# Expert stage of an attention, gated feed-forward and routed-expert kernel: order of the first row turnings, the second gather and the weight splits

## The chip, the cores and the metric

The program runs on one core of a Trainium2 chip, as one launch. The metric is device time in microseconds; lower is better. A profiled execution has a span (first to last instruction) and, a little longer, a time of its own.

## What is computed

Three stages follow one another. Attention makes an array of 1792 tokens x 768 features. A gated feed-forward (`moe_`) maps each token to `(sigmoid(x @ w_gate) * (x @ w_val)) @ w_out`. Then every token goes to one of 8 experts:

```
logits = x @ w_gate                      # 1792 x 8
e_idx = argmax(logits, axis=1)
gate_w = softmax(logits)[n, e_idx]
eom = sigmoid(x @ w_output_gate)
for e in range(8):
    mask = e_idx == e
    h = maximum(x[mask] @ w1[e], 0)      # 768 -> 1024
    out[mask] = gate_w * eom[:, e] * (h @ w2[e])   # 1024 -> 768
```

With these inputs the experts get 254, 262, 211, 264, 216, 255, 174 and 156 tokens, that is 2, 3, 2, 3, 2, 2, 2 and 2 tiles of up to 128 rows: 18 expert tiles, numbered g = 0 to 17. The first tiles of experts 1 to 7 are g = 2, 5, 7, 10, 12, 14 and 16.

## The kernel before

All products are made from 16-bit halves: each number is split into a high part and a low part (the rest), and a product is three passes (high x high, high x low, low x high). ScalarE makes the high part of a weight piece (`split_high`, L815), VectorE the low part (`split_low`, L1042), SyncE loads the raw piece. An expert has 14 pieces: p = 0 to 5 are `w1` (128 x 1024, 512 KB), p = 6 to 13 are `w2` (128 x 768, 384 KB). `w_hi_ready` and `w_lo_ready` count the pieces. Raw pieces go through 7 stage buffers (`stage`), and each load waits until the low part of the piece that used the buffer before has been made; expert 0 has 3 buffers of its own for its first pieces. Split `w1` and `w2` have two homes, for odd and even experts.

**Token stage.** `down(t, s, fs)` (L1449) makes the second product of the feed-forward for token tile t (14 tiles, 12 chunks f, 3 passes, 2 halves of 384 columns: 72 multiplications a tile). ScalarE and VectorE (`y_high` L802, `y_low` L1069) turn the sum into high and low parts, and SyncE stores them to HBM (`store_y`). The routing (L1107 to L1217 on VectorE) runs beside the last two tiles. While it lasts, expert 0's pieces 0 to 5 are split ahead of the first token tile.

**Expert stage.** For tile g GpSimd gathers 128 rows from HBM (`gather`, L602) and TensorE turns them (`turn_rows`, L1493, 12 transposes); VectorE copies them to `x_t` (`rows_out`, L1229). Per tile, TensorE's queue is: the first half of the up product (`up`, b = 0, L1506, 18 multiplications), the 16 transposes of the previous tile's hidden layer (`turn_hidden`, L1515), the second half of `up`, `turn_rows(g + 1)`, and the down product of the previous tile (`rows_down`, L1528, 48 multiplications). ScalarE takes the hidden sums out of PSUM (L848), VectorE splits them (L1244, L1246) and copies the turned hidden layer (`turned_hidden`, L1234); the down product waits for this copy. `rows_done` (L835, ScalarE) weights the result rows and `scatter` (L615) writes them out. Engines take their queues strictly in order and meet at semaphores; the order is written out by hand in `tile(e, s, before, first)` of each engine, where `before` is g - 1 and `first` marks an expert's first tile.

The splits of the next expert's weights stand in the first tile of an expert. ScalarE makes three pieces ahead of that tile's hidden sums, three between them, and the eight `w2` pieces after them. Expert 1 has a catch-up of its own in g = 2. At the seam, `turn_rows(0)` stands behind the last `down`, and GpSimd, after all token tiles are stored, first clears `out_rows`, sends one scatter that writes no row, and then gathers for g = 1.

## Time and profile before

| | us |
|---|---|
| median of 3 runs | 1143.47 |
| lowest and highest run | 1142.17 and 1146.43 |
| profiled execution, its time | 1139.88 |
| profiled execution, its span | 1138.1 |
| TensorE busy | 1100.3 (97% of the span) |
| VectorE, ScalarE, GpSimd busy | 594.7, 425.9, 256.5 |

The token stage's first product starts at 633.22 us of the span, the expert stage's at 804.89, and the last multiplication ends at about 1129.5. The time of the profiled execution lies 3.6 below the median, so differences are added to either, and never an absolute time of the span to the median.

### The profile page before, as it was taken

Reading aid. Unit: us, or ns where it says so; the run is one execution under the profiler, and the core shown is the slowest. Engines: PE = TensorE matmul, PEld = TensorE weight load, DVE = VectorE, ACT = ScalarE, POOL = GpSimd, SP = SyncE. Lnnn points to the kernel's source line nnn. Section 1 sums busy time; section 2 is a strip of 40 time slices with the busy share of each in tenths; the row PEclk is TensorE's granted clock in tenths of the full one; section 3 lists DMA queues with packets and bytes.
Section 4 is the critical chain, followed back from the end, with each engine's and each line's share of the span. In section 5 each row is a group of like instructions: output and inputs, shape, how many; then the busy total and the mean of one; then the engine's idle time right before and its main releaser. Section 6 shows DMA issues by size and latency. Waiting matters only on the chain.

```text
span 1138.1 us, 17823 instructions
## 1 busy us (share of the span) xinstructions
PE 1100.3 (97%) x6617; PEld 573.3 (50%) x6618; DVE 594.7 (52%) x837; ACT 425.9 (37%) x631; POOL 256.5 (23%) x235
## 2 busy tenths in 40 slices
PE   7989999999999999999999999999898999999996
PEld 3434444444455555555555555556454555555554
DVE  7888888887433443333343300015656565556721
ACT  5768777777511111211111200001535253353510
POOL 4756767672200000000000000000211122112211
PEclk9999999999999999999999999999899999999999
DMA  5412222210121111111100501000848355366400
GB/s 144 122 49 62 61 65 58 66 25 17 60 67 56 56 55 55 55 55 55 55 28 1 195 28 41 28 32 23 296 163 319 118 211 206 108 217 225 142 20 18
DMA packets 71978, 104.11 MB, mean 91 GB/s; under 512 B 29310, under 2 KB 47870, under 8 KB 71920
## 3 DMA queue, kind: packets, MB, share of 16 engines
q1 hardware_dynamic: 63680, 89.84, 24.0%
q0 software_dynamic: 3120, 11.02, 2.7%
q10 hardware_dynamic: 5120, 2.48, 0.8%
q8 instruction: 36, 0.59, 0.2%
q14 instruction: 22, 0.18, 0.0%
HBM read 93.88 MB, written 13.76 MB: 95 GB/s over the span
## 4 chain that ended last, share of the span: by engine, by line
PE 87%; ACT 4%; DVE 4%; issue 2%; DMA 2%; ACTq 0%; POOL 0%; DVEq 0%; POOLq 0%; SPq 0%
PE ps L1434 29%; PE ps L1449 15%; PE ps L1528 12%; PE ps L1357 10%; PE ps L1506 7%; PE ps L1336 5%; PE ps L1316 2%; ACT arena L815 2%; DVE arena L1042 2%; PE ps L1348 2%; PE ps L1299 2%; PE ps L1338 1%; DMA arena<-in_moe_w 1%; PE ps L1515 1%; PE ps L1493 1%
## 5 line engine op out<-in xcount | busy, mean ns | idle before, releaser
L1434 PE MATMUL ps<-arena 128*128 128x448 f16 x1728 | 328.8, 352 | 0.0
L1434 PEld LDWEIGHTS ps<-arena 128*128 128x128 f16 x1728 | 168.1, 98 | 155.7
L1449 PE MATMUL ps<-arena 128*128 128x392 f16 (+1 forms) x1008 | 167.3, 329 | 2.4 <-DVE arena L1022 2.4
L1506 PE MATMUL ps<-arena 128*128 128x512 f16 x648 | 150.5, 388 | 5.6 <-DVE arena L1229 5.6
L1042 DVE SCALAR_TENSOR_TENSOR arena<-arena 128x768 f16<-128x768 f32 (+1 forms) x112 | 113.1, 1066 | 74.1 <-ACT arena L815 74.0
L1528 PE MATMUL ps<-arena 128*128 128x384 f16 x864 | 143.3, 326 | 4.0 <-DVE arena L1234 3.6
L1449 PEld LDWEIGHTS ps<-arena 128*128 (+1 forms) x1008 | 98.4, 98 | 70.4 <-DVE arena L1022 2.8
L1357 PE MATMUL ps<-arena 128*128 128x448 f32 x288 | 133.0, 573 | 0.0
L785 ACT ACTIVATE arena<-ps 128x448 f32<-128x448 f32 x48 | 26.1, 543 | 263.0 <-PE ps L1434 263.0
L1016 DVE SCALAR_TENSOR_TENSOR arena<-ps,arena 128x448 f32<-128x448 f32 x48 | 30.0, 624 | 176.0 <-PE ps L1434 96.1
L1528 PEld LDWEIGHTS ps<-arena 128*128 128x128 f16 x864 | 83.5, 98 | 58.6 <-issue 2.5
L940 DVE TENSOR_REDUCE arena<-ps 112x2 f16<-112x896 f32 x96 | 99.2, 1076 | 18.6 <-PE ps L1316 18.5
L815 ACT ACTIVATE arena<-arena 128x768 f16<-128x768 f32 (+1 forms) x112 | 97.5, 929 | 27.6 <-DMA arena<-in_moe_w 23.7
L1506 PEld LDWEIGHTS ps<-arena 128*128 128x128 f16 x648 | 63.7, 100 | 80.1 <-DVE arena L1229 6.4
L712 ACT ACTIVATE arena<-ps,arena 128x896 f32<-128x896 f32 x72 | 72.5, 1007 | 33.3 <-PE ps L1338 33.3
L960 DVE RECIPROCAL arena<-arena 128x448 f32<-128x448 f32 x24 | 70.8, 2951 | 10.3 <-ACT arena L730 10.3
L1336 PE MATMUL ps<-arena 64*128 64x448 f16 (+1 forms) x576 | 72.0, 356 | 3.0 <-ACT arena L712 1.7
L620 POOL MEMSET arena<- 128x1536 f16 x1 | 1.4, 1377 | 324.1 <-PE ps L1434 324.1
L835 ACT ACTIVATE arena<-ps,arena 128x384 f32<-128x384 f32 x36 | 18.9, 576 | 141.4 <-PE ps L1528 141.4
L1357 PEld LDWEIGHTS ps<-arena 128*128 128x128 f32 x288 | 47.6, 191 | 45.5 <-issue 45.5
L802 ACT ACTIVATE arena<-ps 128x768 f16<-128x768 f32 x14 | 11.3, 810 | 144.0 <-PE ps L1449 144.0
L1076 DVE TENSOR_SCALAR arena<-ps 128x16 f32 (+1 forms) x12 | 2.1, 171 | 119.9 <-ACT arena L802 119.9
(170 smaller groups left out, 1078.7 us busy)
## 6 DMA issues: line engine op xcount, KB each, us to landing
arena<-in_moe_w SPq DMA_DIRECT2D x48, 512.0 KB, 6.3
arena<-in_moe_w SPq DMA_DIRECT2D x64, 384.0 KB, 3.9
arena<-in_qk SPq DMA_DIRECT2D x23, 448.0 KB, 3.5
y_parts<-arena SPq DMA_DIRECT2D x16, 384.0 KB, 2.3
arena<-in_v SPq DMA_DIRECT2D x48, 96.0 KB, 2.6
arena<-in_moe_w_out SPq DMA_DIRECT2D x12, 384.0 KB, 5.5
arena<-in_w_out_t SPq DMA_DIRECT2D x11, 384.0 KB, 3.1
arena<-in_moe_w_gate SPq DMA_DIRECT2D x10, 384.0 KB, 4.2
```

The source lines that it names most:

```text
L712: nc.scalar.activation(probs[n % 2][:, :, i - 1], ps_pair(SCORE_SLOT, 128), ACT.Exp, bias=lift[:, 1:2])\
L815: nc.scalar.activation(hi, raw_rows(e, p), ACT.Copy, scale=S_OP).then_inc(w_hi_ready, 1)
L940: nc.vector.tensor_reduce(neg_max[n % 2][:, :, j], ps_pair(max_slot(n, j)), AX_X, ALU.max, negate=True)\
L960: nc.vector.reciprocal(sums_inv[n % 2], sums[n % 2]).then_inc(sums_inv_ready, 1)
L1016: nc.vector.scalar_tensor_tensor(gated[b % 2], ps[:, 2 * (b % 2) + 1, 0:S], 1.0 / S_OP, gate[b % 2], ALU.mult, ALU.mult).then_inc(gated_re ...
L1042: nc.vector.scalar_tensor_tensor(lo, raw_rows(e, p), S_OP, hi, ALU.mult, ALU.subtract).then_inc(w_lo_ready, 1)
L1336: nc.tensor.matmul(outs[h], qk_t[n % 3][rows, 1, kl, ks], qk_t[n % 3][rows, 0, ql], start=(kl + ql == 0), stop=False)
L1357: last = nc.tensor.matmul(ps[:, 6 + h, SQ], v_ones[n % 3][:, c, h * D:h * D + 2 * D], probs[n % 2][:, h, c], start=False, stop=(c == KCH - 1))
L1434: last = nc.tensor.matmul(ps[:, 2 * (b % 2) + g, 0:S], up_w[s][:, g, c, wl], xt[:, b * KC + c, xl], start=(c == 0 and wl + xl == 0), stop= ...
L1449: last = nc.tensor.matmul(ps[:, 4 + 2 * s + h, 0:cols], gt[:, f, gl, bass.ds(t * 128, 128)], wo[:, f, wl, h, 0:cols], start=(f == 0 and gl ...
L1506: last = nc.tensor.matmul(ps[:, b, :], x_t[:, xl, c], w1_s[s][:, c, wl, b * 512:(b + 1) * 512], start=(c == 0 and xl + wl == 0), stop=(c = ...
L1528: last = nc.tensor.matmul(ps[:, 4 + h, 0:HALF_DM], hid_t[:, b, hl, c], w2_s[s][:, k, wl, h * HALF_DM:(h + 1) * HALF_DM], start=(k == 0 and ...
```

## The change

Five things are reordered, and nothing that is computed changes.

1. Seam: the last two chunks of the last `down` are made half by half (`down_half`), and `turn_rows(0)` stands between the halves. ScalarE and VectorE take the halves out one by one, and VectorE's `rows_out(0)` stands ahead of both.
2. GpSimd reads the register that says which stores to wait for earlier, and gathers for g = 1 ahead of the clearing.
3. Weight splits: `w2` pieces of an expert e are split in e's own first tile, four ahead of the hidden sums and four between them, and `w1` of e + 1 behind them. Expert 0's pieces 0 to 10 are split between token tiles, 11 to 13 in g = 0, and expert 1's `w1` in g = 0 (three before, three after the second hidden sum). VectorE's `turned_hidden` of the previous tile now stands behind four low parts of 768 columns, where it stood behind three of 1024.
4. Raw pieces: expert 0 has 2 and then 4 buffers in memory that the feed-forward's first product and its weights have left. Expert 1's fourth load waits until the gather for g = 1 has landed.
5. End: the last down product makes its left half of columns in full and then the right one, in PSUM banks 0 and 1, and each half is weighted and scattered by itself, with indices of half rows.

```diff
@@ SyncE @@
+            sp.wait_ge(gt_lo_ready, B * FC)
+            sp.wait_ge(wo_lo_ready, FC)
...
-            sp.wait_ge(y_sum, TT)
+            sp.wait_ge(y_sum, TT + 1)
             def load_expert(e, s):
-                for p in range(KC + EARLY_STAGES if is_at(e, 0) else 0, PIECES):
+                for p in range(PIECES):
+                    if is_at(e, 1) and p == 3:
+                        sp.wait_ge(gathered, 32)
                     if p >= STAGES:
...
+                        sp.wait_ge(w_lo_ready, PIECES * e + p - STAGES + 1)
+                    elif not is_at(e, 1):
+                        sp.wait_ge(w_lo_ready, PIECES * (e - 1) + p + STAGES + 1)
@@ GpSimd @@
-            pool.wait_ge(route, ROUTE_ROWS)
+            pool.wait_ge(route, ROUTE_FIRST)
             tiles = pool.value_load(counts_i[0:1, 2 * E + 2:2 * E + 3], min_val=2, max_val=TT)
...
+            pool.wait_ge(route, ROUTE_ROWS)
+            pool.wait_ge(y_stored[0], even)
+            pool.wait_ge(y_stored[1], odd)
             gather(0)
             pool.wait_ge(route, ROUTE_DONE)
-            for s in range(2):
-                pool.wait_ge(y_stored[s], 8 * TT)
+            gather(1)
             nc.gpsimd.memset(out_rows, 0.0).then_inc(empty_ready, 1)
...
-            gather(1)
...
-            scatter(last)
+            for h in range(2):
+                cols = slice(h * HALF_DM, (h + 1) * HALF_DM)
+                pool.wait_ge(half_idx_ready, 2)
+                pool.wait_ge(out_ready, rows[h])
+                nc.gpsimd.indirect_dma_start(out=out.rearrange("n (h d) -> (n h) d", h=2),
...
@@ ScalarE @@
-            split_high(0, 0, range(KC))
-            over_token_tiles(act, y_high)
+            split_high(0, 0, (0, 1))
+            y_high(0, 0)
+            split_high(0, 0, (2, 3))
+            y_high(1, 1)
+            split_high(0, 0, (4, 5))
+            y_high(2, 0)
+            split_high(0, 0, range(KC, KC + 4))
+            y_high(3, 1)
+            split_high(0, 0, (KC + 4,))
+            over_token_tiles(act, y_high, 4)
...
             def tile(e, s, before, first):
                 g = before + 1
...
+                if first:
+                    split_high(e, s, range(KC + 5, PIECES) if is_at(g, 0) else range(KC, KC + 4))
+                hidden(g, 0)
                 if is_at(g, 0):
-                    split_high(e + 1, 1 - s, range(KC))
-                else:
+                    split_high(e + 1, 1 - s, range(0, 3))
+                elif first:
+                    split_high(e, s, range(KC + 4, PIECES))
+                hidden(g, 1)
+                if first and not is_at(e, E - 1):
+                    split_high(e + 1, 1 - s, range(3 if is_at(g, 0) else 0, KC))
+                if not is_at(g, 0):
                     rows_done(before)
@@ VectorE @@
             rows_out(0)
-            split_low(0, 0, range(KC, PIECES))
+            for h in range(2):
+                cols = slice(h * HALF_DM, (h + 1) * HALF_DM)
+                dve.wait_ge(y_hi_ready, TT + h)
+                nc.vector.scalar_tensor_tensor(y_parts[1][:, 1, cols], ps[:, 6 + h, 0:HALF_DM], 1.0 / S_OP, y_parts[1][:, 0, cols],
+                                               ALU.mult, ALU.subtract).then_inc(y_lo_ready, 1)
...
+                if first:
+                    split_low(e, s, range(KC + 5, PIECES) if is_at(g, 0) else range(KC, KC + 4))
                 if not is_at(g, 0):
                     turned_hidden(before, 0)
                     turned_hidden(before, 1)
                 hidden_split(g, 0)
...
+                if is_at(g, 0):
+                    split_low(e + 1, 1 - s, range(0, 3))
+                elif first:
+                    split_low(e, s, range(KC + 4, PIECES))
                 rows_out(g + 1)
...
                 hidden_split(g, 1)
...
+                if first and not is_at(e, E - 1):
+                    split_low(e + 1, 1 - s, range(3 if is_at(g, 0) else 0, KC))
@@ TensorE @@
+            def down_half(h):
+                for f in range(FC - 2, FC):
+                    for gl, wl in PASSES:
+                        last = nc.tensor.matmul(ps[:, 6 + h, 0:HALF_DM], gt[:, f, gl, (TT - 1) * 128:TT * 128],
+                                                wo[:, f, wl, h, 0:HALF_DM], start=False, stop=(f == FC - 1 and gl == 1))
+                last.then_inc(y_sum, 1)
+            down(TT - 1, 1, range(4, FC - 2))
+            down_half(0)
             pe.wait_ge(route, ROUTE_DONE)
             turn_rows(0)
+            down_half(1)
             over_experts(pe, tile)
             last = last_tile(pe)
             turn_hidden(last, 0)
             turn_hidden(last, 1)
-            pe.wait_ge(out_ready, 2 * last)
-            rows_down(E - 1, 1, last)
```

TensorE at the seam, before, from the routing table's product to the turning of g = 1:

```order
L1481 MATMUL ps<-arena 128x110 x14
L1449 MATMUL ps<-arena 128x384 x48
L1493 MATMUL ps<-arena 128x128 x12
L386 TENSOR_LOAD arena
L386 ISA x2
L1506 MATMUL ps<-arena 128x512 x36
L1493 MATMUL ps<-arena 128x128 x12
```

TensorE at the same place in the changed kernel (L1526 is `down`, L1628 `down_half`, L1567 `turn_rows`, L1580 `up`):

```order
L1558 MATMUL ps<-arena 128x110 x14
L1526 MATMUL ps<-arena 128x384 x36
L1628 MATMUL ps<-arena 128x384 x6
L1567 MATMUL ps<-arena 128x128 x12
L1628 MATMUL ps<-arena 128x384 x6
L400 TENSOR_LOAD arena
L400 ISA x2
L1580 MATMUL ps<-arena 128x512 x36
L1567 MATMUL ps<-arena 128x128 x12
```

The 12 transposes for g = 0 moved ahead of the last 6 multiplications.

VectorE, first tile of an expert in the loop over experts, before, up to the copy of the next tile's turned rows:

```order
L1042 SCALAR_TENSOR_TENSOR arena<-arena 128x1024 x3
L1233 ISA
L1234 COPY arena<-ps 128x1024
L1233 REGISTER_ALU
L1234 COPY arena<-ps 128x1024
L1243 ISA
L1244 CAST arena<-arena 128x512
L1246 TENSOR_TENSOR arena<-arena 128x512
L1042 SCALAR_TENSOR_TENSOR arena<-arena 128x1024 x3
L1225 REGISTER_ALU
L413 ISA
L1229 COPY arena<-ps 128x768 x2
```

The same in the changed kernel (L1110 is the low part, L1314 `turned_hidden`, L1328 and L1330 the hidden split, L1309 `rows_out`):

```order
L1110 SCALAR_TENSOR_TENSOR arena<-arena 128x768 x4
L1313 ISA
L1314 COPY arena<-ps 128x1024
L1313 REGISTER_ALU
L1314 COPY arena<-ps 128x1024
L1327 ISA
L1328 CAST arena<-arena 128x512
L1330 TENSOR_TENSOR arena<-arena 128x512
L1110 SCALAR_TENSOR_TENSOR arena<-arena 128x768 x4
L1305 REGISTER_ALU
L427 ISA
L1309 COPY arena<-ps 128x768 x2
```

Eight pieces of 768 columns stand where six of 1024 stood; the six of 1024 now end the tile, where eight of 768 did.

## Rows read from the trace of the kernel before

**Rows 1.** The page: span, and busy time of TensorE
```profile
span 1138.1 us, 17823 instructions
PE 1100.3 (97%) x6617; PEld 573.3 (50%) x6618; DVE 594.7 (52%) x837; ACT 425.9 (37%) x631; POOL 256.5 (23%) x235
```
**Rows 2.** Waits of TensorE in the expert stage: total us, times, longest us
```profile
PE ps L1528 <- DVE arena L1234: 3.6, 6, 1.2
```
**Rows 3.** Timeline of TensorE at the seam: start, us, what, [idle before]
```profile
794.11 7.96 PE L1449 MATMUL ps<-arena 128*128 128x384 f16 x48
801.90 0.83 PE L1493 MATMUL ps<-arena 128*128 128x128 f16 x12
804.89 9.63 PE L1506 MATMUL ps<-arena 128*128 128x512 f16 x36 [2.15 <-DVE arena L1229]
816.56 0.84 PE L1493 MATMUL ps<-arena 128*128 128x128 f16 x12 [2.04 <-DMA arena<-y_parts,arena]
818.52 5.75 PE L1506 MATMUL ps<-arena 128*128 128x512 f16 x18 [1.12 <-DVE arena L1229]
```
**Rows 4.** A stretch after a wait: engines' busy time, granted clock, DMA share, GB/s
```profile
806.00:808.00 2.00, 2.00 (x6) 0.76 (x5) 1.44 (x2) 0.20 (x1) 0.77 (x2) 0.50 1.07 309
```
**Rows 5.** Chain of waits at the seam: start, us, what
```profile
804.00 2.68 DMA y_parts<-arena
809.96 6.55 DMA arena<-y_parts,arena
```
**Rows 6.** Gathers: the first one's issue, and landing times of it and all 20
```profile
797.13 1.28 POOL L602 DMA_INDIRECT arena<-y_parts,arena  x1 [0.77 <-POOL arena L591]
DMA to landing us min/median/max: 4.2/4.2/4.2
DMA to landing us min/median/max: 2.2/5.8/7.8
```
**Rows 7.** Timeline of SyncE and ScalarE: first raw `w1` loads, and the third split
```profile
630.85 15.65 SPq L484 DMA_DIRECT2D arena<-in_moe_w  x9
636.82 1.06 ACT L815 ACTIVATE arena<-arena 128x1024 f16<-128x1024 f32 x1 [0.18 <-DMA arena<-in_moe_w]
```
**Rows 8.** Timeline of TensorE: starts in tiles g = 3 to 7
```profile
857.00 5.56 PE L1506 MATMUL ps<-arena 128*128 128x512 f16 x18 [2.36 <-DVE arena L1229]
...
869.22 7.96 PE L1528 MATMUL ps<-arena 128*128 128x384 f16 x48 [1.21 <-DVE arena L1234]
877.02 4.05 PE L1506 MATMUL ps<-arena 128*128 128x512 f16 x18
...
894.15 4.05 PE L1506 MATMUL ps<-arena 128*128 128x512 f16 x18
...
911.28 4.05 PE L1506 MATMUL ps<-arena 128*128 128x512 f16 x18
...
929.06 4.05 PE L1506 MATMUL ps<-arena 128*128 128x512 f16 x18
```
**Rows 9.** Timeline of ScalarE and VectorE in tiles g = 5 and 6
```profile
896.23 2.95 ACT L815 ACTIVATE arena<-arena 128x1024 f16<-128x1024 f32 x3 [0.66 <-issue]
897.32 3.49 DVE L1042 SCALAR_TENSOR_TENSOR arena<-arena 128x1024 f16<-128x1024 f32 x3 [8.59 <-ACT arena L815]
912.60 5.24 ACT L815 ACTIVATE arena<-arena 128x768 f16<-128x768 f32 x7
913.48 7.04 DVE L1042 SCALAR_TENSOR_TENSOR arena<-arena 128x768 f16<-128x768 f32 x8 [5.00 <-ACT arena L815]
920.43 1.28 DVE L1234 COPY arena<-ps 128x1024 f16<-128x1024 f16 x2
```
**Rows 10.** Timeline of the last down product, result copies and scatter
```profile
1121.57 7.97 PE L1528 MATMUL ps<-arena 128*128 128x384 f16 x48 [0.43 <-ACT arena L835]
1130.04 1.05 ACT L835 ACTIVATE arena<-ps,arena 128x384 f32<-128x384 f32 x2 [8.53 <-PE ps L1528]
1131.95 1.00 POOL L615 DMA_INDIRECT out<-arena  x1 [5.57 <-ACT arena L835]
```

More of the change, by code:

```diff
@@ L209, in attention_moe_moe_kernel @@
         slot_w = te(n=TC)
-        EARLY_STAGES = 3
-        early_stage = [ym.take(128, F2, F32) for _ in range(EARLY_STAGES)]
+        EARLY_SPLIT = 5
+        tok = te(n=22)
+        tok_half = [te(U32, 22) for _ in range(2)]
+        half_idx = [ym.take(128, 1, U32) for _ in range(2)]
+        w2_home = [ym.take(128, 2 * DM, F16) for _ in range(EARLY_SPLIT - 1)] + [fixed.take(128, 2 * DM, F16)]
         m2 = Region(gt_at, wst_at)
@@ L224, in attention_moe_moe_kernel @@
         STAGES = 7
+        raw_homes = ((wo_raw_at, fixed_at), (gate_at, gate_end))
+        first_raw = [Region(*home).take(128, F2, F32) for home in raw_homes]
+        next_raw = [Region(home[0] + x * DM * 4, home[1]).take(128, DM, F32) for x in range(2) for home in raw_homes]
         sm = Region(wo_at, fixed_at)
@@ L322, in attention_moe_moe_kernel @@
         w_hi_ready = sem("w_hi_ready")
[L323 removed]
+        first_loaded = [sem(f"first_loaded{p}") for p in range(2)]
+        next_loaded = [sem(f"next_loaded{p}") for p in range(4)]
         w_lo_ready = sem("w_lo_ready")
@@ L825, in _ @@
             y_high(TT - 2, 0)
-            y_high(TT - 1, 1)
-            split_high(0, 0, range(KC, PIECES))
+            for h in range(2):
+                act.wait_ge(y_sum, TT + h)
+                act.wait_ge(y_stored[1], 8 * (TT - 2))
+                nc.scalar.activation(y_parts[1][:, 0, h * HALF_DM:(h + 1) * HALF_DM], ps[:, 6 + h, 0:HALF_DM], ACT.Copy,
+                                     scale=1.0 / S_OP).then_inc(y_hi_ready, 1)
             def rows_done(g):
@@ L836, in rows_done, with hidden @@
                                          scale=slot_w[:, bass.ds(g, 1)]).then_inc(out_ready, 1)
+            def hidden(g, b):
+                act.wait_ge(hid_sum, 2 * g + b + 1)
+                wait(act, hid_lo_ready, 2 * g)
+                nc.scalar.activation(hid[:, b * 512:(b + 1) * 512], ps[:, b, :], ACT.Relu, scale=1.0 / S_OP)\
+                    .then_inc(hid_ready, 1)
             def tile(e, s, before, first):
                 g = before + 1
-                more = first and not is_at(e, E - 1)
@@ L858, in tile @@
+                if not is_at(g, 0):
                     rows_done(before)
-                if more and not is_at(g, 0):
-                    split_high(e + 1, 1 - s, range(KC, PIECES))
             act.wait_ge(route, ROUTE_DONE)
             over_experts(act, tile)
-            rows_done(last_tile(act))
+            last = last_tile(act)
+            ready = [act.to_reg(last + 1 + b) for b in range(2)]
+            for b in range(2):
+                act.wait_ge(half_idx_ready, 2)
+                act.wait_ge(out_sum, ready[b])
+                nc.scalar.activation(out_rows[:, b * HALF_DM:(b + 1) * HALF_DM], ps[:, b, 0:HALF_DM], ACT.Copy,
+                                     scale=slot_w[:, bass.ds(last, 1)]).then_inc(out_ready, 1)
@@ L1218, in _ @@
             assert routed["slot_w"] == ROUTE_DONE, routed
+            stage("tok", nc.vector.tensor_tensor(tok, t5[:, 2], t5[:, 0], ALU.add))
+            need("tok")
+            stage("half", nc.vector.tensor_scalar(tok_half[0], tok, 2.0, None, ALU.mult))
+            stage("half", nc.vector.tensor_scalar(tok_half[1], tok, 2.0, 1.0, ALU.mult, ALU.add))
             y_low(TT - 2, 0)
-            y_low(TT - 1, 1)
             def rows_out(g):
@@ L1250, in tile @@
                 g = before + 1
-                more = first and not is_at(e, E - 1)
-                catch_up = more and is_at(e, 1)
-                if more and not is_at(g, 0) and not catch_up:
-                    split_low(e + 1, 1 - s, range(0, KC // 2))
+                if first:
+                    split_low(e, s, range(KC + 5, PIECES) if is_at(g, 0) else range(KC, KC + 4))
                 if not is_at(g, 0):
@@ L1483, in _ @@
             last.then_inc(route_mm, 1)
-            down(TT - 1, 1, range(4, FC))
             def turn_rows(g):
@@ L1555, in _ @@
             turn_hidden(last, 1)
-            pe.wait_ge(out_ready, 2 * last)
-            rows_down(E - 1, 1, last)
+            pe.wait_ge(w_lo_ready, PIECES * E)
+            for h in range(2):
+                for b in range(2):
+                    if h == 0:
+                        pe.wait_ge(hid_t_ready, 2 * last + b + 1)
+                    for c in range(4):
+                        k = 4 * b + c
+                        for hl, wl in PASSES:
+                            end = nc.tensor.matmul(ps[:, h, 0:HALF_DM], hid_t[:, b, hl, c],
+                                                   w2_s[1][k][:, wl, h * HALF_DM:(h + 1) * HALF_DM],
+                                                   start=(k == 0 and hl + wl == 0), stop=(k == 7 and hl == 1))
+                end.then_inc(out_sum, 1)
 _INS = ["qk", "v", "v_last", "g_qk", "moe_w_gate", "moe_w_val", "moe_w_out", "w_out_t", "moe2_w_gate", "moe2_w_output_gate", "moe2_w1", "moe2_w2"]
```

132 lines of the change are left out of this document (74 added, 58 removed).

## The prediction, made before the changed kernel ran

> **What bounds the kernel now.** The page comes first: TensorE is busy for 1100.3 of 1138.1 us [rows 1], so only its waits, and what it does slowly after them, can be won. They are looked for in TensorE's timeline, from the seam on. The stage in front of it has none that the change touches.
>
> At the seam three waits follow one another [rows 3]: 2.15 us until VectorE has copied the turned rows of g = 0, 2.04 until the gather of g = 1 has landed, and 1.12 until those rows are copied. The chain of waits shows why the gather is late [rows 5]: the last store goes out at 804.00 and lands 2.68 later, but the gather goes out only at 809.96, since the clearing and its scatter stand between. It takes 6.55.
>
> Behind a wait there is a second cost. Between 806 and 808 the granted clock is 0.50, which is 1.2 GHz where 2.4 is full [rows 4], and the 36 multiplications of g = 0 take 9.63 us where two halves at full clock take some 2 x 3.9 [rows 3, 8]. The first half of g = 1 takes 5.75, and that of g = 3 takes 5.56, against 4.05 in an undisturbed tile [rows 3, 8]. A wait of 1.21 us was followed by a down product of the usual 7.96 [rows 8], so short waits don't bring this cost.
>
> In later tiles the starts of the up product are read off [rows 8]: 877.02, 894.15 and 911.28 are 17.13 apart, an undisturbed tile. From g = 6 (911.28) to g = 7 (929.06) it is 17.78, so that tile lost 0.65. The wait there is that of `rows_down` for VectorE's `turned_hidden`; the waits list counts six of this kind, 3.6 us together [rows 2], of which 1.21 is that of g = 3 and five are about 0.48. Rows 9 show the cause. In g = 5 the eight `w2` pieces stand behind everything, so ScalarE makes them in g = 6 (from 912.60), VectorE follows (913.48, eight for 7.04), and only then comes `turned_hidden`, 920.43. Tiles 6, 8, 11, 13 and 15 follow a first tile of experts 2 to 6, which makes the five. In g = 3 the catch-up of expert 1 costs more: 2.36 of wait, and then 20.02 us (857.00 to 877.02) for a tile of 17.13, so 2.36 + 2.89 = 5.25 [rows 8].
>
> **The seam, step by step.** 48 multiplications take 801.90 - 794.11 = 7.79 us [rows 3], 0.162 each. Now 42 stand ahead of the transposes of g = 0: 794.11 + 42 x 0.162 = 800.9. From a turning to the up product it was 818.52 - 816.56 = 1.96 [rows 3], so g = 0 starts at 802.9; the last 6 multiplications (1.0) fit into that time. That is 2.0 earlier than 804.89. It needs the first gather by 800.9. Before, it went out at 797.13 and took 4.2 [rows 6], which gives 801.3; the register read now done earlier should bring about 1 us (it is the nearest estimate of what lay between the index's end and the copy ahead of the gather; the range is 0 to 1, and at 0 everything here is 0.4 later).
>
> With no wait ahead of it, g = 0 runs at full clock and ends its 36 multiplications at 802.9 + 7.8 = 810.7. What follows isn't set by TensorE. The store: it went out 2.1 after the last `down` multiplication (801.90 to 804.00) [rows 3, 5]. Now that ends at 802.6, and only half a result is left to take out, which makes up for the shift; I leave it at 804.0, landing 806.7. The gather follows at once, at 806.8, some 3.2 earlier. It lands between 4.2 (alone) and 7.8 later; I take the median 5.8 [rows 6], so 812.6, and the up product of g = 1 at 812.6 + 1.96 = 814.6, with bounds 813.0 and 816.6.
>
> A second thing is needed there. VectorE now makes three low parts of expert 1's `w1` ahead of the copy of g = 1's rows. In the token stage the third such piece was being split 5.97 after the first load's issue (630.85 to 636.82) [rows 7]. The loads go out at about 804.4, so 810.4, plus the store ahead of them and the gather beside them: each is 384 KB, 1.3 us at 309 GB/s [rows 4]. That gives 811.7 to 813.0. ScalarE's part (1.06) [rows 7], VectorE's (3.49 / 3 = 1.16) [rows 9] and the copy (about 1.1 of the 1.96) bring the start of g = 1 to 815.0 to 816.3. Both paths end within 2 us of each other. I take 815.1, **3.4 us earlier** than 818.52, with bounds of 1.9 (816.6) and 5.5 (813.0). The clearing and the fourth load (held back until the gather lands) are hidden: the first result row copy comes a tile later, and expert 1's weights are needed from g = 2, some 19 us on.
>
> TensorE now waits from 810.7 to 815.1, with 0.8 of transposes between. I take the slow clock in g = 1 at the price that it had, 5.75 - 4.05 = 1.7, so nothing is gained or lost by it. Bounds: no slow clock, 1.7 more gained; all 18 multiplications at 1.2 GHz, twice the 3.9, 2.1 more lost.
>
> The Trainium skill speaks against the step: "DMA: Bandwidth & Descriptors", section "Issuing engines are not separate DMA queues", says that transfers started by SyncE and GpSimd run on the same engines and interleave. By that, the gather isn't ahead of the weight loads merely because it left earlier. The trace agrees: 6.55 us with loads in flight [rows 5], against 4.2 [rows 6]. With 6.55 the start of g = 1 would be 815.3, and the gain 3.2.
>
> **First tiles.** T is the start of a first tile. TensorE's down product starts at T + 17.13 - 7.79 = T + 9.3. ScalarE began its splits at 896.23 in the tile of 894.15, T + 2.1 [rows 8, 9]; four `w2` parts at 5.24 / 7 = 0.75 are made by T + 5.1. VectorE starts 0.9 behind ScalarE [rows 9] and needs 7.04 / 8 = 0.88 each: T + 6.5. `turned_hidden`, two copies in 1.28 [rows 9], ends at T + 7.8, its first at T + 7.2. The margin is 1.5 to 2.1 us, and the second copy has 3.9 more, since the down product takes its half later. The remaining four `w2` parts end at about T + 12.4 behind the hidden split, the copy of the next tile's rows at T + 13.4, needed at T + 17.1. The six `w1` parts (1.16 each) end some 7 us behind a further hidden split, near T + 21.5, which is T' + 4.4 of the next tile. There nothing but the transposes of about T' + 4.9 (4.05 and some 0.9) wants VectorE. ScalarE has done its six (1.06 each) by about T + 16, if the loads keep up: pieces 3 to 5 can be loaded only after the low parts that free their buffers, from T + 9 on, and would land in 6 us. `rows_done` stands behind them and may be 1 or 2 late, which only a scatter sees.
>
> So all waits of rows 2 go: **5 x 0.65 = 3.25 us** and **5.25 us** in g = 3. The work moved is the same in number and size and lies beside TensorE's; if that cover were gone, four low parts (3.5 us) ahead of `turned_hidden` would show, less the margin.
>
> **Token stage.** Splits between token tiles cost nothing: a `down` tile is 72 x 0.162 = 11.7 us, ScalarE's `y_high` and four splits need 4, and the next use of that PSUM buffer is a tile away. If loads were late there, one `y_high` could hold up one tile by a few us; they wait for low parts made a tile before, so I give it nothing.
>
> **The end.** The last down product starts at 1121.57, after 0.43 for the result copy of the tile before [rows 10]. Other banks take that wait away, but `turned_hidden` is needed at nearly the same moment: 0.1. Then one copy of 384 columns is left behind the last multiplication instead of two (1.05 together): 0.5. The scatter went out 1131.95, 0.86 after the copies [rows 10]; the second one of halves does so too. Left half and its scatter lie beside the right half's 24 multiplications (3.9). **0.6 us**, bounds 0 and 1.
>
> **Sum.** 3.4 + 5.25 + 3.25 + 0.6 = 12.5. The profiled execution (1139.88) would become 1127.4. Against the median of the runs, 1143.47, it is 1131.0. I forecast the median of the runs.
>
> **Rivals.** (a) The seam gives nothing: the third `w1` piece or the gather lands so late that g = 1 starts where it did. For it speaks that both paths are within 2 us of each other and that all loads interleave; against it, that the longest of 20 gathers took 7.8. The gain is 12.5 - 3.4 = 9.1: 1134.4. Chance 0.12.
> (b) The wait moves instead of going: `turned_hidden` is late in the first tiles by what the margin lacks. For it: four parts in front, and a `w2` piece that lands late stops them. Against: those pieces are loaded a tile before, and 1.5 us are to spare. At 1 us missed in 7 first tiles: 1138. Chance 0.07.
> (c) Slower than before, by that same place alone: seven first tiles must lose 12.5 / 7 = 1.8 each, so VectorE must end `turned_hidden` 3.3 to 3.9 us later than worked out. A wait over 2 us would bring the slow clock (1.5 to 1.7) with it, which helps it along: 2.4 + 1.6 in each gives 28 lost, 1159. The deciding point is a first `w2` low part at T + 6.5 instead of T + 3. Chance 0.04.
> (d) The change doesn't do what it says at the seam, but more: g = 1 starts by 813.5 and without the slow clock. 12.5 + 1.6 + 1.7: 1127.7. Chance 0.07.
>
> **Numbers.** Forecast 0.70, with 1128.5 to 1133.5 as its own range. 0.5% of the time is 5.7 us, about what a measurement tells from no change, so faster means under 1137.8. Forecast, (a), (d) and part of (b) are faster: 0.90; (b)'s rest is the same: 0.06; slower 0.04. The range takes (a) and most of (d): 1127 to 1136.
>
> **What will show it.** In the changed kernel's TensorE timeline: g = 0 starts 2.0 us after the transposes with no wait ahead of it and 7.8 us for 36; g = 1 starts 12 us after g = 0; all later starts are 17.1 apart; no wait for `turned_hidden` in the waits. On VectorE, `turned_hidden` of first tiles ends before T + 9.3. It is wrong if first tiles show a wait for VectorE, if a token tile waits for `y_low`, or if g = 1 starts more than 14 us after g = 0.

## The result, and the profile after

The changed kernel takes 1130.24 us, the median of four runs (1128.30 to 1130.93). Four runs of the kernel before on the same chip have a median of 1142.82 (1140.79 to 1146.43). The ratio is 0.988, with a 95% interval of 0.9863 to 0.9898. The forecast was 1131.0.

The page of the changed kernel, to be set beside [rows 1]:

```profile
span 1128.2 us, 17810 instructions
PE 1097.2 (97%) x6617; PEld 572.4 (51%) x6618; DVE 595.8 (53%) x841; ACT 428.3 (38%) x632; POOL 252.0 (22%) x237
```

The two spans differ by 9.9 us, but not all of what lies in them belongs to the change. The routing table's product, inside the last `down` tile, starts at 793.40 in the profile of before and at 795.27 in this one, 1.87 later. All of that arose ahead of the token stage, which starts at 633.22 and at 635.08: the token stage itself takes 160.2 up to this product in both profiles, so the splits that now stand between its tiles cost nothing here, as the prediction had it. (In the profiles of experiments 3, 8, 10, 11 and 12 it takes 161.9, without a wait of TensorE in it; no run shows why.) So from here on two measures are used. The **tail** runs from the start of that product to the end of the span: 344.7 us before, 332.93 after, 11.8 gained. And times at the seam are given with a plus sign, as us behind the start of the last `down` product (794.11 before, 795.98 after).

A caution for all tails: the only profile of the kernel before is an execution of 1139.88, below its median in every set of runs (1142.82 to 1144.59). Tail gains against it are smaller than the gains of the medians, by 0.8 here and by up to 4.9 in the experiments. So the whole gain against before is read from the medians, and tails compare the variants of the changed kernel with one another.

TensorE's timeline at the seam of the changed kernel, for [rows 3] (L1558 the table's product, L1526 `down`, L1628 the halves, L1567 the turning of rows, L1580 `up`, L1649 the last product). Its last rows are the starts of g = 2, g = 3 and g = 5 and the last product:

```profile
795.27 0.86 PE L1558 MATMUL ps<-arena 128*128 128x110 f16 x14
795.98 6.01 PE L1526 MATMUL ps<-arena 128*128 128x384 f16 x36
801.82 1.14 PE L1628 MATMUL ps<-arena 128*128 128x384 f16 x6
803.28 0.83 PE L1567 MATMUL ps<-arena 128*128 128x128 f16 x12 [0.32 <-DMA arena<-y_parts,arena]
803.95 1.14 PE L1628 MATMUL ps<-arena 128*128 128x384 f16 x6
805.23 7.94 PE L1580 MATMUL ps<-arena 128*128 128x512 f16 x36
815.76 0.84 PE L1567 MATMUL ps<-arena 128*128 128x128 f16 x12 [2.59 <-DMA arena<-y_parts,arena]
818.33 5.75 PE L1580 MATMUL ps<-arena 128*128 128x512 f16 x18 [1.73 <-DVE arena L1309]
...
837.16 4.05 PE L1580 MATMUL ps<-arena 128*128 128x512 f16 x18
...
854.30 4.05 PE L1580 MATMUL ps<-arena 128*128 128x512 f16 x18
...
888.56 4.05 PE L1580 MATMUL ps<-arena 128*128 128x512 f16 x18
...
1112.78 7.96 PE L1649 MATMUL ps<-arena 128*128 128x384 f16 x48 [0.43 <-DVE arena L1314]
```

g = 0 now starts at +9.25, with no wait but the 0.32 ahead of its transposes (before +10.78, 1.5 later) and runs at full clock, 7.94 for 36 instead of 9.63. But g = 1 starts at +22.35 (before +24.41): only 2.06 earlier, and its first half is as slow as before, 5.75. In place of one wait ahead of g = 0 and two ahead of g = 1, TensorE waits 2.59 and 1.73 on the two sides of the transposes of g = 1. The granted clock there, as in [rows 4] (PE, PEld, DVE, ACT, POOL, clock, DMA share, GB/s):

```profile
818.00:820.00 2.00, 1.67 (x5) 0.68 (x6) 1.40 (x3) 0.72 (x1) 0.48 (x1) 0.63 1.01 406
820.00:822.00 2.00, 2.00 (x7) 0.64 (x6) 1.57 (x2) 1.56 (x3) 0.00 (x0) 0.52 1.02 411
```

The chain of waits there, for [rows 5], and GpSimd's gathers, for [rows 6]:

```profile
797.49 5.66 DMA arena<-y_parts,arena
...
804.15 1.02 DVE arena L1309 x2
805.17 0.46 DVE arena L1321
...
806.28 0.34 SPq L518
...
807.65 7.35 DMA arena<-in_moe_w
...
815.03 1.06 ACT arena L869
...
817.26 1.02 DVE arena L1309 x2
```

```profile
797.49 1.28 POOL L639 DMA_INDIRECT arena<-y_parts,arena  x1 [0.30 <-POOL arena L628]
...
809.77 1.02 POOL L639 DMA_INDIRECT arena<-y_parts,arena  x1 [6.31 <-DMA y_parts<-arena]
```

The first gather leaves at +1.51 instead of +3.02, but takes 5.7 instead of 4.2. The second leaves at +13.79 instead of +15.85 and takes 6.0. It waits for the last store, which leaves at +10.30 (before +9.89) and lands 2.7 later, as before; from that landing to the gather's issue another 0.8 passes.

Two things in this chain are easily overlooked. The store is late because of the reorder itself: VectorE now copies the rows of g = 0 (L1309) ahead of the last halves (L1321), so the store, and the weight loads behind it in SyncE's queue, wait for the first gather. And what TensorE waits for last, ahead of g = 1, is not the gather but the third `w1` load: it lands at 815.0, ScalarE makes its high part in 1.06, VectorE the low part, and only at 817.26 the copy of g = 1's rows starts. The gather lands at 815.8, so the two paths end within a microsecond of each other.

TensorE's waits from the seam on show that nothing of [rows 2] is left:

```profile
PE ps L1567 <- DMA arena<-y_parts,arena: 2.9, 2, 2.6
PE ps L1580 <- DVE arena L1309: 1.7, 1, 1.7
PE ps L1649 <- DVE arena L1314: 0.4, 1, 0.4
```

ScalarE and VectorE in the first tile g = 5, which starts at 888.56, for [rows 9]:

```profile
890.55 3.05 ACT L869 ACTIVATE arena<-arena 128x768 f16<-128x768 f32 x4 [0.56 <-issue]
891.43 3.56 DVE L1110 SCALAR_TENSOR_TENSOR arena<-arena 128x768 f16<-128x768 f32 x4 [8.29 <-ACT arena L869]
894.91 1.28 DVE L1314 COPY arena<-ps 128x1024 f16<-128x1024 f16 x2
```

With T = 888.56, the four low parts end at T + 6.4 and `turned_hidden` at T + 7.6; the prediction had 6.5 and 7.8. From the start of g = 2 to the last turning of a hidden half, 282.74 us before became 274.14: **8.6 gained** in tiles 2 to 17.

The end, for [rows 10]:

```profile
1118.16 0.58 ACT L931 ACTIVATE arena<-ps,arena 128x384 f32<-128x384 f32 x1 [5.43 <-POOL arena L689]
1120.84 0.58 ACT L931 ACTIVATE arena<-ps,arena 128x384 f32<-128x384 f32 x1 [2.11 <-PE ps L1649]
1122.21 0.98 POOL L694 DMA_INDIRECT out<-arena  x1 [1.65 <-ACT arena L931]
```

From the last product's start to the scatter's issue it is 9.43 instead of 10.38, 0.95 less.

### The profile page after: what moved, and what is told of

Read it like the earlier page. It is cut to its first block, busy times and chain, and to the rows that moved or that the text cites. A ratio compares the mean times of both kernels' runs of the same rounds, so it can differ in the third digit from the quotient of the medians.

```text
span 1128.2 us, 17810 instructions
## 1 busy us (share of the span) xinstructions
PE 1097.2 (97%) x6617; PEld 572.4 (51%) x6618; DVE 595.8 (53%) x841; ACT 428.3 (38%) x632; POOL 252.0 (22%) x237
## 4 chain that ended last, share of the span: by engine, by line
PE 93%; ACT 2%; DVE 2%; DMA 1%; issue 1%; ACTq 0%; POOL 0%; SPq 0%; DVEq 0%; POOLq 0%
PE ps L1511 29%; PE ps L1526 14%; PE ps L1580 12%; PE ps L1602 12%; PE ps L1434 10%; PE ps L1413 5%; PE ps L1393 2%; PE ps L1425 2%; PE ps L1376 2%; PE ps L1415 1%; PE ps L1589 1%; PE ps L1567 1%; PE ps L1649 1%; DMA arena<-in_moe_w 1%; ACT arena L763 1%
## 5 line engine op out<-in xcount | busy, mean ns | idle before, releaser
L1511 PEld LDWEIGHTS ps<-arena 128*128 128x128 f16 x1728 | 168.1, 98 | 155.7
L1526 PE MATMUL ps<-arena 128*128 128x392 f16 (+1 forms) x996 | 165.3, 329 | 2.4 <-DVE arena L1090 2.4
L1110 DVE SCALAR_TENSOR_TENSOR arena<-arena 128x768 f16<-128x768 f32 (+1 forms) x112 | 113.3, 1066 | 67.9 <-ACT arena L869 67.7
L1580 PE MATMUL ps<-arena 128*128 128x512 f16 x648 | 147.3, 382 | 1.9 <-DVE arena L1309 1.7
L1602 PE MATMUL ps<-arena 128*128 128x384 f16 x816 | 135.4, 326 | 0.0
L1526 PEld LDWEIGHTS ps<-arena 128*128 (+1 forms) x996 | 97.2, 98 | 69.6 <-DVE arena L1090 2.8
L1602 PEld LDWEIGHTS ps<-arena 128*128 128x128 f16 x816 | 79.1, 98 | 50.6
L1580 PEld LDWEIGHTS ps<-arena 128*128 128x128 f16 x648 | 62.9, 98 | 74.0 <-DVE arena L1309 2.4
L566 POOL TENSOR_TENSOR arena<-arena 112x16 f32<-112x16 f32 x21 | 60.9, 2902 | 1.8
```

Of the source, the lines that this page charges most:

```text
L566: nc.gpsimd.tensor_tensor(rms_inv, rms_sq, minus_half, ALU.pow).then_inc(rms_inv_ready, 1)
L1110: nc.vector.scalar_tensor_tensor(lo, raw_rows(e, p), S_OP, hi, ALU.mult, ALU.subtract).then_inc(w_lo_ready, 1)
L1511: last = nc.tensor.matmul(ps[:, 2 * (b % 2) + g, 0:S], up_w[s][:, g, c, wl], xt[:, b * KC + c, xl], start=(c == 0 and wl + xl == 0), stop= ...
L1526: last = nc.tensor.matmul(ps[:, 4 + 2 * s + h, 0:cols], gt[:, f, gl, bass.ds(t * 128, 128)], wo[:, f, wl, h, 0:cols], start=(f == 0 and gl ...
L1580: last = nc.tensor.matmul(ps[:, b, :], x_t[:, xl, c], w1_s[s][:, c, wl, b * 512:(b + 1) * 512], start=(c == 0 and xl + wl == 0), stop=(c = ...
L1602: last = nc.tensor.matmul(ps[:, 4 + h, 0:HALF_DM], hid_t[:, b, hl, c], w2_s[s][k][:, wl, h * HALF_DM:(h + 1) * HALF_DM], start=(k == 0 and ...
```

## The experiments

Two questions stand behind them. The first: did the reordered seam (half products, gather ahead of the clearing) give the gain at g = 1? The rival is that the reorder gives nothing, and that g = 1 is earlier because the five `w2` loads and eight splits of expert 0 left the seam, so the gather has less company. The second: is it the parts ahead of `turned_hidden` that decide the first tiles, with 1.5 us or a little more to spare, or does their number not matter? Ratios are to the kernel before on the same chip. Where no ratio stands, there was one run of the kernel, beside one of before at 1143.96. "Start of g = 1" and "g = 2" are us behind the last `down` product's start.

**1. Only the splits moved.** Against the changed kernel; seam and end as before.

```diff
-            down(TT - 1, 1, range(4, FC - 2))
-            down_half(0)
+            down(TT - 1, 1, range(4, FC))
             turn_rows(0)
-            down_half(1)
...
+            gather(1)
             def tile(e, s, before, first):
```

> The changed kernel with the old seam (whole last down product, then the transposes of g = 0; gather of g = 1 behind the clearing) and the old end; only the weight splits and raw buffers are new. I measure the tail: from the start of the routing table's product to the end of the span, 344.7 us before and 332.9 in the changed kernel. Theory (the split order alone removes the waits for turned_hidden and the catch-up, 8.5 us, and the seam and the end give 2.1 and 1.1 by themselves): no wait of TensorE in tiles 2 to 17, tail 336 us, time 8 to 9 us under the kernel before. Rival (the parts lean on each other: the new splits need the earlier seam, else expert 1's pieces come late): a wait of 1 us or more in g = 2 or 3, and less than 6 us gained.

Measured: 1130.52, ratio 0.988 (0.9855 to 0.9906), tail 332.65. TensorE at the seam:

```profile
803.15 0.83 PE L1540 MATMUL ps<-arena 128*128 128x128 f16 x12
806.14 9.63 PE L1553 MATMUL ps<-arena 128*128 128x512 f16 x36 [2.15 <-DVE arena L1286]
815.79 0.84 PE L1540 MATMUL ps<-arena 128*128 128x128 f16 x12
818.23 4.06 PE L1553 MATMUL ps<-arena 128*128 128x512 f16 x18 [1.59 <-DVE arena L1286]
```

Within the intervals, some 3 us wide on either side, this is the whole gain; the expectation had only 8 to 9 us and a tail of 336. g = 0 still waits 2.15 and is slow, 9.63. But the gather, though it leaves 2.7 later than in the changed kernel (+16.48), has landed when g = 0 ends, and no slow half follows. g = 1 starts at +22.88, g = 2 at +40.02, where the changed kernel has +22.35 and +41.18. The new end, which this kernel lacks, makes up for the difference in the tail.

**2. Only the seam reordered,** on the kernel before, with its splits.

```diff
+            down(TT - 1, 1, range(4, FC - 2))
+            down_half(0)
             pe.wait_ge(route, ROUTE_DONE)
             turn_rows(0)
+            down_half(1)
...
             pool.wait_ge(route, ROUTE_DONE)
-            for s in range(2):
-                pool.wait_ge(y_stored[s], 8 * TT)
+            gather(1)
```

> The kernel before with only the new seam (half products around the transposes of g = 0, gather of g = 1 ahead of the clearing). Theory: the seam is worth 2 us by itself, as measured between the two kernels (g = 1 starts 22.4 us behind the last down product's 48 multiplications instead of 24.4), and the waits of the later tiles stay, 8.5 us of them; tail 342 to 343 us. Rival (expert 0's eight w2 pieces, which stand in front of the copy of g = 1's rows here, hold g = 1): gain under 1 us, tail 344 or more.

Measured: 1141.65 against 1144.59, ratio 0.9972 (0.9961 to 0.9984), tail 344.9 (before 344.7). TensorE:

```profile
806.23 7.94 PE L1513 MATMUL ps<-arena 128*128 128x512 f16 x36
817.95 1.46 PE L1500 MATMUL ps<-arena 128*128 128x128 f16 x12 [3.78 <-DMA arena<-y_parts,arena]
820.77 6.88 PE L1513 MATMUL ps<-arena 128*128 128x512 f16 x18 [1.36 <-DVE arena L1234]
```

The gather left at 810.79 and landed 7.1 later, beside the `w2` loads. What was won ahead of g = 1 (it starts at +23.77) is lost to a slower clock: g = 2 starts at +43.73, before at +43.24. The profile has the tail of before, as the rival expected. But it is of the slowest of the seven runs, 1143.03, set against the execution of before that lies below its median. The timed runs, whose interval is clear of 1, say 0.28%, about 3 us. So beside the `w2` loads the reorder alone gives between 1.8 and 4.5 us in the medians; no profile shows where, and that stays open.

**3 and 4. More `w2` parts ahead of `turned_hidden`:** eight, and six, where the changed kernel has four. The edit for eight, on ScalarE; VectorE has the same for `split_low`, and six has KC + 6:

```diff
-                    split_high(e, s, range(KC + 5, PIECES) if is_at(g, 0) else range(KC, KC + 4))
+                    split_high(e, s, range(KC + 5, PIECES) if is_at(g, 0) else range(KC, KC + 8))
...
-                    split_high(e, s, range(KC + 4, PIECES))
+                    split_high(e, s, range(KC + 8, PIECES))
```

> The changed kernel with all eight w2 splits of a first tile (experts 1 to 7) ahead of the hidden sums and of turned_hidden, instead of four and four. Theory (the margin of turned_hidden is 1.5 to 2.1 us, and each low part costs 0.88): VectorE would end eight at T + 10.0 and the first copy at T + 10.7, so the down product waits 1.3 us beyond T + 9.3 in each of 7 first tiles, up to 9 us in all, 11 to 20 if the slow clock joins in; time 1138 to 1142. Rival (the copy is not what the down product waits for, ScalarE or the loads set it): no wait, time as in the changed kernel.

> As the one with eight ahead, but with six: VectorE ends them at T + 8.2 and the first copy at T + 8.9, inside T + 9.3. Theory: no wait for turned_hidden, or at most 0.2 us in a tile; time within 1 us of the changed kernel. Rival (any longer queue ahead of turned_hidden costs in proportion): half of what eight cost.

Measured: eight, 1136.58, ratio 0.9936 (0.9916 to 0.9956), tail 341.63; six, 1129.59, ratio 0.9877 (0.9855 to 0.9899), tail 333.0, with no wait for `turned_hidden`. The wait of eight, in the list of waits, and one of them on VectorE:

```profile
PE ps L1602 <- DVE arena L1314: 7.2, 7, 1.4
```

```profile
892.70 7.04 DVE L1110 SCALAR_TENSOR_TENSOR arena<-arena 128x768 f16<-128x768 f32 x8 [8.28 <-ACT arena L869]
899.66 1.28 DVE L1314 COPY arena<-ps 128x1024 f16<-128x1024 f16 x2
```

Eight low parts hold up the seven first tiles by 1.0 each (1.3 were expected, and 1138 us or more). Six, with 2 x 0.88 more than four, still fit. So the margin is between 1.8 and 3.5 us; with 1.0 missed at four parts more, it is about 3.5 - 1.0 = 2.5, where 1.5 to 2.1 was worked out. That `turned_hidden` decides the first tiles is shown. These waits, 0.8 to 1.45 us long, brought no slow clock: every down product after them took 7.96.

**5 and 6. Fewer splits, then fewer loads ahead of g = 1.** In 5 the three `w1` splits stand behind the copy of g = 1's rows. 6 is 5 and also holds back all `w1` loads but the first until the gather has landed.

```diff
-                if is_at(g, 0):
-                    split_low(e + 1, 1 - s, range(0, 3))
...
-                    if is_at(e, 1) and p == 3:
+                    if is_at(e, 1) and p == 1:        # in 6 only
                         sp.wait_ge(gathered, 32)
```

> The changed kernel, but in g = 0 the three w1 splits of expert 1 that stood ahead of the second hidden sum and of the copy of g = 1's rows stand behind them, on ScalarE and VectorE. In the changed kernel the gather landed at the start of the transposes, 19.8 us behind the last down product's start, and g = 1 began 22.35 behind it, 2.57 after the transposes, of which 1.96 is the way from a turning to an up product. Theory (the third w1 piece costs the remaining 0.6, the gather the rest): g = 1 starts 21.7 to 21.8 behind, 0.6 us earlier. Rival (w1 alone sets it): 1.5 us or more earlier.

> As e5, and of expert 1's raw loads only the first goes out before the gather of g = 1 has landed (before: three). Theory (the gather took 6.0 us instead of 4.2 because three loads of 512 KB run beside it): it lands 1 to 1.8 us earlier and g = 1 starts 20 to 21 us behind the last down product's start. Rival (the gather's time is its own or the store's): landing as before, nothing gained. Risk: the held pieces come late, and turned_hidden in g = 1 or the up product of g = 2 waits.

Measured: 5, 1127.38, tail 330.45, g = 1 at +21.58; 6, 1125.09, tail 329.8, g = 1 at +19.29. TensorE in 6:

```profile
811.55 0.84 PE L1563 MATMUL ps<-arena 128*128 128x128 f16 x12 [0.59 <-DMA arena<-y_parts,arena]
813.51 4.06 PE L1576 MATMUL ps<-arena 128*128 128x512 f16 x18 [1.11 <-DVE arena L1307]
...
824.49 7.96 PE L1598 MATMUL ps<-arena 128*128 128x384 f16 x48 [1.48 <-DVE arena L1312]
```

The loads are what delays the gather: with one beside it, it lands in 3.9 (807.61 to 811.5) instead of 6.0. But of the 2.3 by which g = 1 starts earlier than in 5, most comes back a tile later, as 1.48 for `turned_hidden`, because the held loads bring their splits into g = 1: g = 2 is at +38.07, against +38.73 in 5. In 5 g = 1 starts 0.8 earlier than in the changed kernel; 0.6 of that is what the splits had cost, as expected: the wait behind the transposes is 1.12 instead of 1.73, since the copy no longer stands behind the third load. Its gather is as slow as in the changed kernel (a wait of 2.52), yet the half after it runs at full clock, 4.06, which was not expected and makes up the rest of the tail's 2.5. So the wait isn't enough to tell whether the slow clock follows.

**7. The wait filled.** TensorE runs 11 and 7 multiplications on a constant, whose result nothing reads, where it waited.

```diff
                 up(e, s, g, 1, first)
+                if is_at(g, 0):
+                    idle_work(11)
                 turn_rows(g + 1)
+                if is_at(g, 0):
+                    idle_work(7)
```

> The changed kernel with multiplications without use (11 ahead of the transposes of g = 1, 7 behind them, into a free PSUM bank) where TensorE waits. Theory (the slow clock follows the wait): the granted clock stays at 1.00, the first half of g = 1's up product takes 4.05 us instead of 5.75, and everything behind comes 1.7 us earlier, tail 331.2. Rival (the up product is slow for another reason, its operands or PSUM): 5.75 as before.

Measured: 1128.51, tail 330.44. TensorE, then the clock:

```profile
816.94 1.67 PE L1367 MATMUL ps<-arena 128*128 128x512 f16 x7
818.60 4.06 PE L1585 MATMUL ps<-arena 128*128 128x512 f16 x18
```

```profile
816.00:818.00 2.00, 1.90 (x18) 1.17 (x18) 1.98 (x4) 0.83 (x2) 0.26 (x2) 1.00 0.25 66
818.00:820.00 2.00, 2.00 (x10) 0.80 (x9) 1.57 (x4) 0.03 (x1) 0.99 (x1) 1.00 0.96 391
```

The clock stays at 1.00, and the half takes 4.06 instead of 5.75. So the 1.7 was the clock's and not the data's. The other 0.8 of the tail's 2.5 is not the fill's: g = 1 started at +21.53, since the first gather landed in 5.3 here and the store left 0.5 earlier. This is one execution, and 1, 5, 6 and 11 kept the full clock there without a fill. For the fill speaks that all five profiles with the changed kernel's seam and its loads unaltered (the changed kernel, 3, 4, 8 and 10) have the slow half, 5.71 to 5.92.

**8. The store of token tile 12 held until the first gather has landed.**

```diff
+            sp.wait_ge(gathered, 16)
             store_y(TT - 2, 0)
```

> The changed kernel, but the store of token tile 12 waits until the gather of g = 0 has landed (that gather needs only the first token tiles here). Theory (the gather of g = 0 went out 1.5 us earlier than before but landed no earlier, 5.7 us instead of 4.2, because it now meets this store): it lands in 4.2 or less, the wait of 0.32 us ahead of the transposes of g = 0 goes, and g = 0 starts 0.3 to 0.5 earlier; g = 1 moves by no more than that, or is held if the store is late. Rival: 5.7 as before, it is the gather's own time.

Measured: 1131.02, tail 333.2. The transposes of g = 0 come at +6.83 instead of +7.30 and wait for nothing, and the first gather takes 5.0 instead of 5.7. The expectation was 4.2 or less, so the store is at most a part of it. Even that part isn't shown: in 6, 7 and 12, where the store is not held, the transposes also come at +6.82 to +6.90, with a gather of 5.3 to 5.4. Nor does before, with 4.2, speak for it, since there a store had left 1.0 ahead of the gather and was in flight too. Why the first gather takes longer when it leaves earlier stays open. g = 0 starts 0.47 earlier, but g = 1 at +22.49, as in the changed kernel.

**9 to 12. Combined and taken apart, on one chip.** 9 has the splits of 5, two loads ahead of the gather and a fill of 4 and 4. 12 is 9 without the fill. 10 is the changed kernel again. 11 is the changed kernel with the last `down` product whole again, ahead of the turning, and with ScalarE and VectorE taking its result out whole, ahead of the copy of g = 0's rows:

```diff
-            down(TT - 1, 1, range(4, FC - 2))
-            down_half(0)
+            down(TT - 1, 1, range(4, FC))
             pe.wait_ge(route, ROUTE_DONE)
             turn_rows(0)
-            down_half(1)
```

> The changed kernel with expert 1's w1 splits behind the rows of g = 1 (as e5), two raw loads instead of one ahead of the gather's landing (e6 had one, and then 1.48 us of wait for turned_hidden in g = 1), and 4 multiplications without use ahead of and 4 behind the transposes of g = 1. Theory (the seam is now set by the gather, the loads beside it and the slow clock): g = 1 starts about 20 us behind the last down product's start (22.35 in the changed kernel), at full clock, no wait in g = 1; tail 329 us against 332.9, time 3 to 4 us under the changed kernel. Rival (the loads held back come late wherever the line is drawn): 1 us or more of wait in tile 1 or 2, tail 330 or more.

> The changed kernel once more, as measure for the other three of this call. Tail about 333 us; g = 1 starts 22.4 behind the last down product's start. Both theories expect the ratio to the kernel before that it had, 0.988.

> The changed kernel with the old seam on TensorE (whole last down product, then the transposes of g = 0), but with the gather of g = 1 ahead of the clearing and the new end. Theory (the wait ahead of g = 0 takes the slow clock there, where it is hidden behind the gather, and the half products bring nothing): g = 1 starts 22 to 22.5 behind, at full clock, g = 2 at 39.2 to 40 (41.18 in the changed kernel), tail 331 to 332. Rival (the half products are worth the 1.5 us by which g = 0 starts earlier): tail 334 or more.

> As e9 without the multiplications without use. Theory (the waits left, about 1 us each side of the transposes, are too short to bring the slow clock): the same as e9 within 0.5 us. Rival (the clock falls in some executions): up to 1.7 us more, and a first half of g = 1's up product of 5 to 6 us.

| | median (runs) | ratio, 95% | tail | g = 1 | g = 2 |
|---|---|---|---|---|---|
| 9 combined | 1127.04 (1126.44 to 1129.00) | 0.9849 (0.9831 to 0.9868) | 329.93 | +20.78 | +38.22 |
| 10 changed | 1131.02 (1128.34 to 1131.43) | 0.9873 (0.9850 to 0.9896) | 333.43 | +22.93 | +41.72 |
| 11 product whole | 1126.79 (1126.21 to 1129.22) | 0.9847 (0.9828 to 0.9866) | 330.45 | +21.31 | +38.46 |
| 12 not filled | 1126.62 (1126.41 to 1128.92) | 0.9846 (0.9827 to 0.9865) | 330.45 | +20.24 | +38.67 |

TensorE in 11:

```profile
795.45 7.96 PE L1518 MATMUL ps<-arena 128*128 128x384 f16 x48
803.25 0.83 PE L1559 MATMUL ps<-arena 128*128 128x128 f16 x12
806.24 7.94 PE L1572 MATMUL ps<-arena 128*128 128x512 f16 x36 [2.15 <-DVE arena L1305]
814.10 0.84 PE L1559 MATMUL ps<-arena 128*128 128x128 f16 x12
816.76 4.06 PE L1572 MATMUL ps<-arena 128*128 128x512 f16 x18 [1.82 <-DVE arena L1305]
```

The same 2.15 ahead of g = 0 as in the kernel before, but at full clock after it, where the expectation had the slow clock there and g = 1 at +22 or later. TensorE isn't there before the gather has landed (it went out at +14.11 and took 4.5), and one wait of 1.82 remains. Against 10, g = 1 starts 1.6 earlier and its first half runs 1.65 faster (5.71 there): together 3.3, a little more than the 3.0 between the tails. The medians are 4.2 apart, though the intervals overlap.

The store and the loads no longer wait for the first gather in 11: the first `w1` load leaves at +10.27, against +10.69 in the changed kernel and +11.08 in 10. So the loads are 3.8 ahead of the gather instead of 3.1, and the gather lands at +18.6 instead of +19.8, though it left 0.3 later.

12 has shorter waits than the changed kernel, 1.49 and 1.12, and still a slow half, 5.34, as its rival had it; in time it is level with 9, as its theory had it. 9 has waits of 0.66 and 0.25 left and no slow half. Its gather, with two loads beside it, took 4.9, and g = 1 started 0.8 later than was expected.

All of 9, 11 and 12 have a lower median than both kernels. 11 is the plainest of them: it takes one part of the change back. Its combination with the splits of 5 wasn't tried.

## Why the prediction was right, and where it was wrong

**The sum** was 12.5. The medians differ by 12.6 and the tails by 11.8; 1131.0 against 1130.24 is 0.1% off. It was right in total: one term held, and two erred in opposite directions. That they nearly cancel is luck. Worked out again from the traces the terms are 2.1, 8.6 and 0.95, 11.6 together. The seam's 2.1 rests on the one profile of before, which lies below its median; from the medians 12.6 - 8.6 - 0.95 = 3.0 would be left for it.

**First tiles, 8.5: right,** 8.6 measured. The cause that [rows 9] gave is shown by 3 and 4. Of the costs, T + 6.5 and T + 7.8 were 6.4 and 7.6. The margin was larger than worked out, about 2.5. Rival (b) needed four parts to be too many; even six aren't. Its price of 1 us for each first tile is what eight cost.

**The end, 0.6: too small,** 0.95. The half copy gave 0.5 as worked out, and it starts 0.1 us after the last multiplication instead of 0.5. The 0.43 of wait stayed, with VectorE as its releaser in place of ScalarE.

**The seam, 3.4: mis-sized and put down to the wrong part.** The steps, one by one:
- "g = 0 starts at 802.9", 2.0 earlier: 1.5. The first gather left 1.5 earlier (0 to 1 was the range) but landed no sooner, at +7.2 in both, having taken 5.7 instead of 4.2. The prediction took the 4.2 as that of a gather alone, but a store was in flight beside it. What stretched it isn't shown.
- "I leave it at 804.0, landing 806.7": the store took the 2.7 that it had, but left 0.4 later, since the copy of g = 0's rows now stands ahead of the halves. "The gather follows at once, at 806.8" was wrong: it left 0.8 after the landing. Together it came out 1.1 late; relative to the same start it would have been 807.9.
- "I take the median 5.8": 6.0.
- "That gives 811.7 to 813.0" for the third `w1` load: it landed at 815.0, relative to the same start 813.1, just past the late end. By its own sum that path gave 815.0 to 816.3 for g = 1, and 815.1 was taken, nearly its early end; 816.5 was measured. This path, and not the gather's, ended last.
- "Short waits don't bring this cost", from one wait of 1.21: in 12, after 1.49 and 1.12, they did, 5.34.
- "I take the slow clock in g = 1 at the price that it had": it was there, 5.75. Together g = 1 is 2.06 earlier and g = 2 also 2.06.

The step that failed behind these is the assumption that the reorder on TensorE and GpSimd, by an earlier gather, is what moves g = 1. Experiment 1, without the reorder, has the same time and tail. Experiment 2, with it alone, gains about 3 us in the medians, but on top of the new splits the same reorder adds nothing that the runs show. What helped was that the `w2` loads and splits of expert 0 left the seam, a part that the prediction had costed only for the later tiles. In experiment 1 the gather left 2.7 later than in the changed kernel and landed only 0.6 later. The landing goes with the loads in flight: 6.0 with three loads in front, 4.9 with two, 3.9 with one, 7.1 with the `w2` loads. The sentence weighed in the prediction, from the Trainium skill's "DMA: Bandwidth & Descriptors", section "Issuing engines are not separate DMA queues", says that transfers of different issuing engines run on the same DMA engines and interleave; these traces agree with it. Rival (a), a seam that gives nothing, was right about the reorder once the splits had moved, and wrong about the seam as a whole.

That the split product even costs something is what 11 suggests, 4.2 us in the medians and 3.0 in the tail. How much of it is the order and how much the chance of the clock isn't settled: the clock's part is 1.65 in these two profiles.

**Sign and range.** Of the signs that were named, g = 0 without a wait of its own, no wait for `turned_hidden` ahead of the last product, and later starts 17.1 apart were borne out. One was not: g = 1 came 13.1 after g = 0, not 12, within the 14 that would have refuted it.

## What to carry to other kernels

A transfer that is sent earlier into the same company of loads may land hardly earlier (here 2.7 us earlier brought 0.6); count the bytes that are in flight between its issue and its landing, and take those away first. When a copy is pulled ahead in an engine's queue, look at what now stands behind it: here it held up the last store and all loads that follow the store. And test a change of several parts by running each part alone, since a total that agrees with the forecast can come from another part than the one it was credited to.

## What the runs showed of the hardware

- A gather of 384 KB landed in 3.9, 4.9 and 6.0 us with one, two and three weight loads of 512 KB issued ahead of it, the first of them 3.1 to 3.2 us ahead, and in 7.1 beside `w2` loads. With three loads it was 5.8 to 6.4 in seven kernels where the first load had left 3.1 to 3.2 us ahead, but 4.5 where it had left 3.8 ahead (11) and 3.9 where it had left 6.2 ahead (1).
- The same waits are not always followed by 1.2 GHz. After 2.15 us ahead of g = 0 the 36 multiplications took 9.63 us in the kernel before and in experiment 1, and 7.94 in 11. After 2.52 and 1.12 the half took 4.06 (5), after 1.49 and 1.12 it took 5.34 (12, at a granted clock of 0.50 between 816 and 818), and after 2.59 and 1.73 it took 5.75 (changed). Where the waits were filled with work, wholly in 7 and for the most part in 9, it took 4.06. No run tells what separates the others.
